# Second layer of a fused attention and two-layer feed-forward kernel: its second product written as seven block products for eight, and its first product made three pairs ahead in four banks

## The reference

```python
# 32 heads of 576 x 64, block-causal softmax attention -> x [2304, 512]
h = x @ w_in1; g = piecewise square of h; x2 = g @ w_out1     # 512 -> 2048 -> 512
h = x2 @ w_in2; g = h * cos(h);           out = g @ w_out2
```

## Time and profile before

| | us |
|---|---|
| median of 3 runs (1042.15 to 1044.34) | 1043.65 |
| the profiled execution | 1051.79 |
| its span, first to last instruction | 1049.6 |
| PE busy in it | 1001.9 (95%) |
| DVE / ACT / POOL busy | 657.0 / 590.8 / 426.5 |

### The profile page before, as it was taken

How to read it: one execution, slowest core, us unless ns; L and a number is a source line. 1 busy time by engine, 2 the same in 40 slices (tenths; PEclk the granted TensorE clock), 3 DMA queues, 4 the chain that set the end, 5 groups by cost and what they waited for, 6 DMA issues and landing times.

```text
span 1049.6 us, 19879 instructions
## 1 busy us (share of the span) xinstructions
PE 1001.9 (95%) x7360; PEld 943.1 (90%) x7360; DVE 657.0 (63%) x1422; ACT 590.8 (56%) x1232; POOL 426.5 (41%) x446
## 2 busy tenths in 40 slices
PE   4688999999999999999999999999999999999997
PEld 3578999999999999999999998999999999999995
DVE  5567777766766767666732378656565555656553
ACT  5567776766666666666633356544444444445442
POOL 3559765555555554655522221222222222222211
PEclk9579999999999999999999999999999999999999
DMA  4335321221211212121200144010110101001000
GB/s 133 104 118 157 98 90 65 72 70 49 92 49 53 89 49 72 70 72 65 69 31 22 41 161 162 1 40 0 40 40 0 40 0 40 21 19 40 0 21 21
DMA packets 30886, 62.28 MB, mean 59 GB/s; under 512 B 3680, under 2 KB 11872, under 8 KB 30816
## 3 DMA queue, kind: packets, MB, share of 16 engines
q1 hardware_dynamic: 29664, 57.16, 17.1%
q10 hardware_dynamic: 1152, 4.19, 1.1%
HBM read 51.90 MB, written 9.44 MB: 58 GB/s over the span
## 4 chain that ended last, share of the span: by engine, by line
PE 79%; DVE 9%; ACT 5%; issue 3%; POOL 1%; DMA 1%; ACTq 0%; POOLq 0%; DVEq 0%
PE hidden L1090 33%; PE acc L1107 18%; PE acc L1115 12%; PE heads_out L1036 4%; PE scores L1001 4%; PE turned L1019 3%; PE scores L1002 3%; DVE neg_max L800 1%; PE heads_out L1019 1%; DVE x_lo L879 1%; PE hidden L1073 1%; DVE wout_lo L865 1%; DVE work L885 1%; ACT probs L616 1%; DVE pt_lo L817 1%
## 5 line engine op out<-in xcount | busy, mean ns | idle before, releaser
L543 POOL TENSOR_TENSOR g_lo<-work,g_hi 128x512 fp32r<-128x512 f32 x144 | 187.9, 1305 | 450.7 <-ACT g_hi L713 450.7
L1090 PE MATMUL hidden<-x_hi,win_hi 128*128 128x256 f32 x1136 | 323.5, 285 | 2.8 <-DVE work L912 1.2
L1090 PE MATMUL hidden<-x_hi,win_lo 128*128 128x256 f32 x1136 | 317.9, 280 | 0.0
L1090 PE MATMUL hidden<-x_lo,win_hi 128*128 128x256 f32 x1136 | 317.9, 280 | 0.0
L1090 PEld LDWEIGHTS hidden<-x_hi,win_hi 128*128 128x128 f32 x1136 | 214.3, 189 | 7.6 <-issue 2.0
L1090 PEld LDWEIGHTS hidden<-x_lo,win_hi 128*128 128x128 f32 x1136 | 214.2, 189 | 3.3
L1090 PEld LDWEIGHTS hidden<-x_hi,win_lo 128*128 128x128 f32 x1136 | 216.4, 190 | 0.0
L1115 PE MATMUL acc<-g_hi,wout_hi 128*128 128x256 f32 x576 | 167.4, 291 | 0.3 <-ACT y_stage L696 0.3
L1115 PE MATMUL acc<-g_lo,wout_hi 128*128 128x256 f32 x576 | 160.6, 279 | 0.0
L1115 PE MATMUL acc<-g_hi,wout_lo 128*128 128x256 f32 x576 | 160.5, 279 | 0.0
L513 POOL TENSOR_SCALAR probs<-probs,row_inv 64x576 f32<-64x576 f32 (+2 forms) x160 | 107.4, 675 | 121.6 <-DVE row_inv L812 120.8
(11 more groups left out here) (91 smaller groups left out, 1830.1 us busy)
## 6 DMA issues: line engine op xcount, KB each, us to landing
qk_raw<-qk_late SPq DMA_DIRECT2D x32, 448.0 KB, 3.2
qk_raw<-qk_early SPq DMA_DIRECT2D x32, 256.0 KB, 2.6
v_raw<-v_late SPq DMA_DIRECT2D x32, 160.0 KB, 3.3
x_raw<-x_scratch SPq DMA_DIRECT2D x9, 512.0 KB, 3.5
out<-y_stage SPq DMA_DIRECT2D x36, 128.0 KB, 2.4
x_raw<-w_in SPq DMA_DIRECT2D x8, 512.0 KB, 3.6
y_stage<-w_out SPq DMA_DIRECT2D x8, 512.0 KB, 3.5
x_scratch<-y_stage ACTq DMA_DIRECT2D x8, 512.0 KB, 2.7
```

Source lines behind the costliest of these rows:

```text
L543: nc.gpsimd.tensor_tensor(g_lo[:, m % G_RING, :], work[:, m % 2, :], g_hi[:, m % G_RING, :], ALU.subtract).then_inc(g_lo_made, 1)
L1090: last = nc.tensor.matmul(into, w[:, p, c, half * P:(half + 1) * P], x[:, c, :], start=(i == 0), stop=(i == len(products) - 1))
```

## The change

Take a pair's g as 2 x 2 blocks (two halves of the channels, two halves of the tokens, 128 x 128 each) and its w_out as 2 x 2 blocks of 128 x 256. The product is made by a form of Strassen's scheme: four sums of g blocks, four sums of w_out blocks, seven block products instead of eight, added over the pairs in seven half banks of PSUM, and put together once per tile. With three parts each this is 21 matmuls of 256 columns.

* The sums of w_out (`weight_sums`, POOL, four per pair) are made in tiles 6 and 7, at the eight places `BLOCKS_AT`, and go to DRAM (`t_dram`) and back. The three plain blocks are split there as well (`split_blocks`: ACT, then DVE) and stay in `w_parts`.
* The sums of g (`sum_blocks`) are three more DVE operations per pair that read SBUF twice: 256, 128 and 128 columns. ACT's high part is now 384 columns of plain blocks (`blocks_hi`) and 512 of sums (`sums_hi`); POOL's low part the same (`blocks_lo`, `sums_lo`).
* `read_acc` of the second layer becomes `move_p1` (ACT) and `combine` (five DVE operations).
* The first product is made three pairs ahead (`SECOND_LAG`), in four banks (`hidden` and `acc`). g's buffers hold two pairs. There is one buffer of `turns` and one of `sums`.
* Pair 7's first product goes through the channels of x in both rows, so x's first half is free in its middle (`x_used`). `split_x` has two parts, placed apart.
* In the first layer `G_RING` is 3 instead of 4. Three of the second layer's weight pieces are split in tile 9, which is now written out.

```diff
+SECOND_LAG = 3
+BLOCKS_AT = [divmod((TILES - 3) * UNITS + 24 + 5 * pair, UNITS) for pair in range(PAIRS)]
...
+            def use_blocks(t, p):
...
+                products = {1: (p1, 0, 0), 2: (p2, 2, 1), 4: (p4, 1, 5), 3: (p3, 6, 2), 5: (p5, 4, 4), 6: (p6, 5, 6), 7: (p7, 3, 3)}
+                order = (6, 7, 1, 5, 2, 3, 4) if p == 0 else (1, 2, 4, 3, 5, 6, 7)
+                pe.wait_ge(g_lo_made, PAIRS * t + p + 1 + 2)
+                for k in order:
+                    into, g_block, w_block = products[k]
+                    if k == (6 if p == 0 else 3):
+                        pe.wait_ge(sums_lo_made, PAIRS * (t - TILES) + p + 2)
+                    if p == 0 and k in (6, 1, 2, 4):
+                        pe.wait_ge(y_part, 5 * (t - TILES) + {6: 2, 1: 3, 2: 4, 4: 5}[k])
+                    g = [g_blocks(p, low)[:, g_block * P:(g_block + 1) * P] for low in range(2)]
+                    for part, (left, right) in enumerate(((g[0], w_hi), (g[1], w_hi), (g[0], w_lo))):
+                        last = nc.tensor.matmul(into, left, right[w_block],
...
# ACT
+            def blocks_hi(t, m):
+                act.wait_ge(hidden_read, PAIRS * t + m + 1 + H_BANKS)
+                act.wait_ge(g_used, PAIRS * t + m - 1 + G_RING)
...
+            def second_tile(t, next_tile=True, last_weights=False):
+                for s in range(PAIRS):
+                    m = s + SECOND_LAG
+                    if m == PAIRS - 1 and next_tile:
+                        split_x(t + 1, True, 1)
+                        sums_hi(t, m - 2)
+                    if m < PAIRS or next_tile:
+                        round_turns(t, m)
+                    if s == PAIRS - 1:
+                        move_p1(t)
+                    if m - 1 < PAIRS or next_tile:
+                        blocks_hi(t, m - 1)
+                    if m < PAIRS or next_tile:
+                        cosine(t, m)
+                    if m == PAIRS - 2 and next_tile:
+                        split_x(t + 1, True, 0)
+                    elif m - 1 < PAIRS or next_tile:
+                        sums_hi(t, m - 1)
...
# DVE
+            def sum_blocks(t, m):
...
+                nc.vector.tensor_tensor(sums[:, 0:2 * P].rearrange("p (b n) -> p b n", b=2),
...
+                nc.vector.tensor_tensor(sums[:, 2 * P:3 * P], sums[:, P:2 * P], g[1], ALU.subtract).then_inc(sum_part, 1)
+                dve.wait_ge(sum_part, 2 * count)
+                nc.vector.tensor_tensor(sums[:, 3 * P:4 * P], g[3], sums[:, 2 * P:3 * P], ALU.add).then_inc(sums_made, 1)
+            def combine(t):
+                done = 5 * (t - TILES) + 5
+                dve.wait_ge(p1_moved, t - TILES + 1)
+                nc.vector.tensor_tensor(y[3], y[3], p6, ALU.subtract).then_inc(y_part, 1)
+                dve.wait_ge(y_part, done + 1)
+                nc.vector.tensor_tensor(y_blocks[:, 0:2, :], twice(y[3]), twice(p7), ALU.add).then_inc(y_part, 1)
...
+            def second_tile(t, next_tile=True, last_weights=False):
+                for s in range(PAIRS):
+                    m = s + SECOND_LAG
+                    if m == PAIRS - 1 and next_tile:
+                        split_x(t + 1, True, 0)
+                        split_x(t + 1, True, 1)
+                    if m < PAIRS or next_tile:
+                        angle(t, m)
+                    if s == PAIRS - 1:
+                        combine(t)
+                    if m - 1 < PAIRS or next_tile:
+                        sum_blocks(t, m - 1)
+                    if m < PAIRS or next_tile:
+                        times_cosine(t, m)
...
# PE
+                    if m < PAIRS or next_tile:
+                        make_hidden(t, m, 0, leading=True)
+                        make_hidden(t, m, 1, leading=True)
...
+                    use_blocks(t, s)
```

More of the change, by code:

```diff
@@ L27 @@
 LAG = 2
-G_RING = 4
+G_RING = 3
 H_BANKS = 2
@@ L464, in load_second @@
[L464 to L473, removed]
+                    src = (w2_in, t_dram)[which][pair, :, h * 512:(h + 1) * 512]
@@ new lines, in load_second @@
+                    sp.dma_start(stage_second[which][h], src).then_inc(half_in[which][h], 16)
+            load_blocks(0)
+            load_blocks(1)
+            for pair in range(PAIRS):
+                store_t(pair)
+                if pair + 2 < PAIRS:
+                    load_blocks(pair + 2)
+                if pair == PAIRS - 2:
+                    sp.wait_ge(x_lo_made, x_pieces_by(TILES - 1))
+                    sp.wait_ge(y_stored, 16 * 2)
+                    load_x2(0)
+            for pair in range(PAIRS):
@@ L763, in replace_wout, with lead @@
                 split_second(1, pair)
+            def second_tile(t, next_tile=True, last_weights=False):
[16 more added lines that the diff above has]
+                        sums_hi(t, m - 1)
+                    if last_weights and s == 0:
+                        split_second(0, PAIRS - 1)
+                    if last_weights and s in (1, 5):
+                        replace_wout(PAIRS - 2 + s // 5)
+            def lead():
+                m = SECOND_LAG - 1
+                round_turns(TILES, m)
+                blocks_hi(TILES, m - 1)
+                cosine(TILES, m)
+                sums_hi(TILES, m - 1)
             split_k_hi(0)
@@ L778, in _ @@
             tile(TILES - 1, to_second=True)
-            replace_wout(PAIRS - 1)
-            with act.Fori(TILES, 2 * TILES - 1) as t:
-                tile(t, second=True)
-            tile(2 * TILES - 1, second=True, next_tile=False)
+            lead()
+            second_tile(TILES, last_weights=True)
+            with act.Fori(TILES + 1, 2 * TILES - 1) as t:
+                second_tile(t)
+            second_tile(2 * TILES - 1, next_tile=False)
         @block.vector
@@ L916, in tile @@
+            def tile(t, beside=None, to_second=False):
                 made_in = slots_made(beside is not None)
@@ L975, in _ @@
             tile(TILES - 1, to_second=True)
[L976 to L979 removed]
+            lead()
+            second_tile(TILES, last_weights=True)
+            with dve.Fori(TILES + 1, 2 * TILES - 1) as t:
+                second_tile(t)
+            second_tile(2 * TILES - 1, next_tile=False)
         @block.tensor
@@ L1089, in make_hidden @@
                         pe.wait_ge(x_lo_made, x_pieces_by(t + m // PAIRS) - (0 if i else 1))
-                    last = nc.tensor.matmul(into, w[:, p, c, half * P:(half + 1) * P], x[:, c, :],
-                                            start=(i == 0), stop=(i == len(products) - 1))
+                    into = bank[:, rows * TOK:(rows + 1) * TOK]
+                    last = nc.tensor.matmul(into, w[:, p, c, rows * P:(rows + 1) * P], x[:, c, :],
+                                            start=(i == 0 and (half == 0 or not split)),
+                                            stop=(i == len(products) - 1), skip_group_check=True)
@@ new lines, in use_hidden @@
+                for d in range(KC):
+                    if d == KC // 2:
+                        beside_half(beside, 2 * u)
+                    into = acc[:, d // 2, (d % 2) * TOK:(d % 2 + 1) * TOK]
+                    for part, (w, g) in enumerate(((wout_hi, g_hi), (wout_hi, g_lo), (wout_lo, g_hi))):
+                        last = nc.tensor.matmul(into, w[:, p, half, d * P:(d + 1) * P],
+                                                g(i)[:, half * TOK:(half + 1) * TOK],
+                                                start=(p == 0 and half == 0 and part == 0 and d % 2 == 0),
+                                                stop=(p == PAIRS - 1 and half == 1 and part == 2), skip_group_check=True)
+                    if i == PAIRS * TILES - 1 and half == 1 and d == 1:
+                        last.then_inc(acc_made, 1)
@@ L1119, in use_hidden, with blocks @@
                 if half == 1:
                     last.then_inc(g_used, 1)
-            def tile(t, beside=None, second=False, to_second=False, next_tile=True):
+            def use_blocks(t, p):
+                def blocks(low):
+                    t_blocks = whole_of((wout_hi, wout_lo)[low], p)
+                    return ([w_blocks(p, low)[:, b * WBLOCK:(b + 1) * WBLOCK] for b in range(3)]
+                            + [t_blocks[:, b * WBLOCK:(b + 1) * WBLOCK] for b in range(4)])
+                w_hi, w_lo = blocks(0), blocks(1)
+                products = {1: (p1, 0, 0), 2: (p2, 2, 1), 4: (p4, 1, 5), 3: (p3, 6, 2), 5: (p5, 4, 4), 6: (p6, 5, 6), 7: (p7, 3, 3)}
[10 more added lines that the diff above has]
+                        last = nc.tensor.matmul(into, left, right[w_block],
+                                                start=(p == 0 and k in (6, 1, 2, 4) and part == 0),
+                                                stop=(p == PAIRS - 1 and part == 2), skip_group_check=True)
+                last.then_inc(g_used, 1)
@@ L1159, in _ @@
             tile(TILES - 1, to_second=True)
-            with pe.Fori(TILES, 2 * TILES - 1) as t:
-                tile(t, second=True)
```

(10 more changed lines are left out.)

451 lines of the change are left out of this document (277 added, 174 removed).

## The result

| | before | changed |
|---|---|---|
| median of 4 runs, us | 1043.99 (1042.15 to 1044.58) | 1068.47 (1067.88 to 1069.43) |
| ratio, 95% interval | | 1.0238 (1.0221 to 1.0256) |
| the profiled execution / its span | 1051.79 / 1049.6 | 1068.84 / 1067.0 |

The account below looks back on a forecast made before the run. PE bounds the second layer before; afterwards the ACT-DVE ring: 8 x 5.23 + 1.3 + 2.55 = 45.7 us a tile. Span 1063.5, 13.9 above 1049.6, added to the median: 1057.5; its own range 1046 to 1070, overall 1027 to 1075.

Parts of the forecast that it names:

- The ring: Second layer, closed chain round, angle, abs, sine, sums_hi, next round over ACT and DVE: about 5.23 us a step.
- rival 1: In the second layer's angle, L896 doesn't wait for POOL: ring 4.95, time about 1041 us; chance 0.22.
- Rival 3: L896 loses the lock twice, also to blocks_lo: ring 6.2, tile 53, above 1110 us; with weaker forms chance 0.08.
- Once a tile: Second layer: x pieces add 1.3 us and combine 2.55 to eight ring steps, making a tile 45.7.
- The step with combine: At s = 7, combine stands between angle(10) and sum_blocks(9) on DVE: +2.55 us a tile.
- the x step: At m = 7, ACT's two x pieces between sine(6) and round(7), with sums_lo's delay: 1.3 us a tile.
- the difference goes onto the median: Span forecast 1063.5, 13.9 above 1049.6; this difference added to the median 1043.65 gives 1057.5 us.
- Round(3): Start of the second layer's ring count, after the first layer ends at 644.4: forecast at 653.2 us.
- two signs of being wrong: Tile period under 44.7, or tile period right but first layer or change of layers moved by more than 3 us.
- Tiles 6 and 7 "0": First layer: the weight sums there fit where POOL, ACT and DVE have room, costing 0, or a few us once.
- Tile 9: Three weight pairs split there, 1.2 us of DVE each: +3.6 us on the ring, 45.7 + 3.6.
- Rival 2: PE stays the second layer's bound, at a ring of 4.83 us or less: about 1025 us; chance 0.15.

Follow-up runs that it names:

- the first variant: Changed kernel with ACT making sums_hi of pair m-2 right behind round(m), POOL's order following: 1037.75 us, ratio 0.9935 to the kernel before; run again 1038.55 us.
- e2: Changed kernel with POOL's sums_lo making 64 of its 512 columns, order untouched: 1038.43 us, ratio 0.9936 to the kernel before.
- e5: Apparently the changed kernel with POOL's four w_out sum operations per pair cut from 256 columns to 4: 1066.76 us, ratio 1.0203 to the kernel before.
- e6: The first variant with the eight places of the w_out sums moved out of the last units before a tile's copy: 1040.02 us, ratio 0.9952 to the kernel before.
- e8: Changed kernel with the first product waiting until the pair three back is read, not four, so three banks in use: 1066.63 us, ratio 1.0213.
- the second variant: Changed kernel with ACT making sums_hi(m-2) behind blocks_hi(m-1), and blocks_lo before sums_lo on POOL: 1062.99 us, ratio 1.018 to the kernel before.

## Why the prediction was right, and where its numbers were off

Where the 25.0 us between the spans 1042.0 (second trace of before) and 1067.0 lie, from the starts of the copies into `y_stage`; the last column is the first variant:

| stretch | before | changed | | first variant |
|---|---|---|---|---|
| to the copy of tile 7 | 597.8 | 603.2 | +5.4 | 601.6 |
| tile 8 | 45.9 | 46.3 | +0.4 | 47.1 |
| tile 9 | 44.6 | 54.7 | +10.1 | 46.1 |
| tiles 10 to 17 | 347.9 | 354.7 | +6.8 | 331.8 |
| from the last copy to the end | 5.8 | 8.1 | +2.3 | 8.1 |

* **The ring.** Forecast 5.23, measured 5.13. L1069 waits as predicted: its end comes 0.28 us after that of sums_lo, in every tile of the loop. That puts out rival 1, in which it stays at 0.43. L1075 was thought to wait for blocks_lo; it doesn't, since blocks_lo ends (809.15) just as it starts (809.10), and it keeps its 0.69. That is the missing 0.1. Rival 3 is out too: L1069 does not lose the lock to blocks_lo, it is blocks_lo that gets longer (1.21 us here, 1.01 beside the short sums_lo of e2). The Trainium skill, SBUF — State Buffer, section "Who interferes with whom", says that a tensor_scalar in a 2-port mode and GpSimd block each other; the trace now agrees, 1.06 us beside sums_lo and 0.43 without.
* **Once a tile.** The step with combine is 7.67 (L1069 from 794.30 to 801.97), 2.54 over an ordinary one, forecast 2.55; the x step 6.16 (817.47 to 823.63), 1.0 over, forecast 1.3. Tile 44.87, forecast 45.7. PE stands 2.4 us in it, as forecast, but more of that in front of combine than in front of x. The lines of the combine step:

```profile
794.30 1.06 DVE L1069 TENSOR_SCALAR probs<-probs 128x512 f32<-128x512 f32 x1 [0.40 <-ACT probs L849]
...
796.19 0.69 DVE L1075 SCALAR_TENSOR_TENSOR work<-probs,work 128x512 f32<-128x512 f32 x1
796.80 0.41 DVE L1112 TENSOR_TENSOR y_stage<-y_stage,banks 128x256 f32<-128x256 f32 x1
797.24 0.69 DVE L1114 TENSOR_TENSOR y_stage<-y_stage,banks 128x512 f32<-128x512 f32 x1
797.97 0.69 DVE L1117 TENSOR_TENSOR y_stage<-y_stage,banks 128x512 f32<-128x512 f32 x1
798.69 0.69 DVE L1119 TENSOR_TENSOR y_stage<-y_stage,banks 128x512 f32<-128x512 f32 x1
799.29 0.41 DVE L1120 TENSOR_TENSOR y_stage<-y_stage,banks 128x256 f32<-128x256 f32 x1
799.62 0.42 DVE L1099 TENSOR_TENSOR probs<-work 128x256 f32<-128x256 f32 x1
```

* **The step that failed: "the difference goes onto the median".** The span was forecast at 1063.5 and came at 1067.0, only 3.5 off; the median is 11 off. The other 7.5 is the base. The profiled execution before had the slow rhythm in a layer bound by PE: 5.59 us a pair instead of 5.49, 7 us over 72 pairs. The changed kernel is bound by the ring and the rhythm hardly reaches its time: in its loop tiles some first products have 0.114 us a matmul and some 0.118, every tile takes 44.8 to 44.9, and its profiled execution (1068.84) is its median. The right base for the tile was 43.9, not 44.7.
* **Where it was luck.** Part of the agreement is luck. The span came within 3.5 because misses of both signs cancel. Round(3) starts at 659.67, forecast 653.2: 6.5 late, by the first layer, the wait for y_stage and the half-speed product behind it. Tile 9 takes 51.6 (to 711.25) for 49.3. Seven loop tiles take 0.84 less each than forecast, 5.9 together. In the same way the forecast of 1.0 us more per tile came close (0.9) with both tiles forecast 0.8 too long. And of the 25.0 us only 6.8 lie in tiles 10 to 17, which the ring with its once-a-tile terms was worked out for; 15.5 lie in the first layer and tile 9. The prediction's last paragraph names two signs of being wrong. The tile period stayed above 44.7, barely; but the first layer and the change of layers both moved by more than 3 us, so by its own sign it was wrong there, though its direction, its ring and its range held.
* **Tiles 6 and 7 "0".** Not borne out: the first layer is 5.4 us late against the second trace of before. Of this, 3.1 are there at the copy of tile 5, before any weight sum (497.8 against 494.7); e5 and the first variant, with the same first layer, had that copy at 496.4 and 496.0, so about half of the 3.1 comes and goes between executions. Tiles 6 and 7 together take 105.4 for 103.1. A wait of 0.9 us for y_stage, which before had not, is the change's, and the moved places of e6 take it away; in tile 6 the 256-column matmuls come every 0.117 us on average for 0.115. Whether that rhythm is the change's isn't settled.
* **Tile 9.** From round(3) to round(11) it takes 51.6, 6.7 over a loop tile; forecast +3.6 for the weight pieces. All three pieces of DVE meet POOL and take 1.98 us for their two operations (L1034), where the first variant has 1.28, and the first product of pair 8 came at half speed, 1.8 us more. The product of pair 2, just ahead of this stretch, did too: below.
* **Rival 2** had the right point of decision. It named a ring of 4.83 us or less; e2's is 4.57, and the tile fell to 42.1. The first variant's fell to 42.2. Its argument was the three pairs of lead; in the changed kernel one bank less costs nothing (e8), so there the lead is not what decides.

## What to carry to other kernels

When the bound engine gets less work, write down the closed ring of waits of the others, in program order, and compare its length to the new period; lead doesn't shorten it (e8), and a single buffer can close another ring when the order changes (`sums` in the second variant). An operation with nothing after it on the path (here a rounding copy) can still be inside a ring, because of what is queued behind it. A forecast added to a median needs a profiled execution that is like the median. A total that comes close says little until its terms are compared one by one.

## What the runs showed of the hardware

* **Two rhythms of matmuls at a granted clock of 1.00:** 256 columns every 0.113 us or every 0.118. First-layer tiles without attention showed either, in the same kernel and without a wait of PE between (the first variant went from 2.72 to 2.83 for 24 at 590 us; traced a second time, it had 0.118 throughout tile 7). What chooses isn't known. Of the 43 timed executions of the kernel before beside the experiments, six took 1050.0 to 1052.5 us and 37 took 1042.3 to 1045.6; two executions of it were traced, one of each kind. Both traces of the first variant have 0.118 in the loop tiles, where the usual execution of before has 0.114; three traces don't say whether that is the kernel's doing.
* **The clock's lower level after a short wait.** In the changed kernel PE waited 1.95 us until 650.46, and from 651.4 on the matmuls of 256 columns came every 0.213 us, which is 1.2 GHz, for 3.2 us. The timeline there:

```profile
650.46 0.36 PE L1325 MATMUL acc<-x_hi,win_hi 128*128 128x256 f32 x1 [1.95 <-DVE y_stage L1086]
...
651.59 0.42 PE L1325 MATMUL acc<-x_hi,win_lo 128*128 128x256 f32 x1
651.80 0.41 PE L1325 MATMUL acc<-x_hi,win_hi 128*128 128x256 f32 x1
```

The windows view of the same ten microseconds, where the granted clock is the third number from the end, 0.83:

```profile
650.00:660.00 10.00, 9.54 (x69) 9.57 (x70) 5.81 (x13) 4.83 (x9) 2.46 (x3) 0.83 0.13 54
```

It happened again at the waits of 2.95 us before 685.28, of 2.28 before 707.97 and of 2.35 before 1053.02; behind the waits of the loop tiles, up to 1.5 us, the granted clock stayed at 1.00. The length of the wait alone doesn't tell: at the same place as the first, the second variant waited 2.01 us and the first variant, traced again, 1.91, and both kept 1.00. Where it happened, the 24 matmuls at 650.46 and at 685.28 took 4.59 and 4.60 us instead of 2.83, so the wait cost itself and some 1.8 us more:

```profile
650.46 4.59 PE acc L1325 x24
...
685.28 4.60 PE hidden L1325 x24
```
